# Decayed keys and normalised rows turned on VectorE and by transfers, in place of TensorE

## The reference

```
f = 1 / (1 + exp(-f_logit))
for t in range(S):
    state = f[t, :, None] * state + outer(k[t], v[t])
    y[t] = q[t] @ state
x = y as 3072 rows of 384
xn = x / sqrt(mean(x * x) + 1e-6) * rms_g
x = (silu(xn @ w_gate) * (xn @ w_val)) @ w_out         # hidden width 1536
h = x @ w_in                                           # hidden width 2048
g = h if h >= 1; 0 if h <= -1; else (h + 1)^2 / 4
out = g @ w_out2
```

## Time and profile before

| | |
|---|---|
| median of 3 runs | 984.48 us (984.31 to 984.51) |
| profiled execution | 984.23 us, span 982.5 us |
| busy: TensorE, its weight load, VectorE, ScalarE, GpSimd | 966.8, 943.4, 585.9, 341.8, 22.4 us |
| chain that ended last | TensorE 95%, VectorE 3%, issue 1% |
| slices of the span at a granted clock below 0.9 | none |
| transfers | 42.32 MB in 15774 packets |

### The profile page before, as it was taken

One profiled execution on the slowest core, in us unless ns is written; L12 is line 12 of the kernel. 1 busy time (PEld: TensorE's weight loads), 2 busy tenths in 40 slices (PEclk: granted clock), 3 DMA queues, 4 the chain that ended last, 5 costly groups with the idle time before them and its releaser, 6 DMA issues.

```text
span 982.5 us, 20662 instructions
## 1 busy us (share of the span) xinstructions
PE 966.8 (98%) x8227; PEld 943.4 (96%) x8227; DVE 585.9 (60%) x1196; ACT 341.8 (35%) x624; POOL 22.4 (2%) x58
## 2 busy tenths in 40 slices
PE   6899999999999999999999999999999999999998
PEld 6899999999999999999999999999999999999998
DVE  8778665574674765665565565555545554545454
ACT  2343322322322222223224454344344344434433
POOL 0100000000000000000000000000000000000000
PEclk9999999999999999999999999999999999999999
DMA  5541111011120110111120400000000000000000
GB/s 194 190 149 43 40 42 50 32 48 40 40 71 9 61 52 13 68 40 40 40 87 17 136 27 1 25 0 24 0 24 0 24 0 19 5 5 19 0 25 25
DMA packets 15774, 42.32 MB, mean 43 GB/s; under 512 B 1408, under 2 KB 8064, under 8 KB 15744
## 3 DMA queue, kind: packets, MB, share of 16 engines
q1 hardware_dynamic: 15744, 41.88, 12.5%
HBM read 37.16 MB, written 4.72 MB: 43 GB/s over the span
## 4 chain that ended last, share of the span: by engine, by line
PE 95%; DVE 3%; issue 1%; POOL 0%; ACT 0%; DMA 0%; DVEq 0%; POOLq 0%
PE gate_ps L403 15%; PE val_ps L403 15%; PE acc L479 13%; PE gate_ps L467 10%; PE val_ps L467 10%; PE acc L425 10%; PE acc L483 7%; PE acc L429 5%; PE tb L314 2%; PE y_ps L338 2%; PE y_ps L344 2%; PE tb L324 1%; DVE qd L721 1%; PE ta L300 1%; DVE after L700 1%
## 5 line engine op out<-in xcount | busy, mean ns | idle before, releaser
L837 DVE TENSOR_TENSOR h_lo<-h_buf,h_hi 128x384 fp32r<-128x384 f32 x224 | 123.3, 551 | 13.2 <-ACT h_hi L648 6.2
L641 ACT ACTIVATE act_buf<-act_buf,half_col 128x384 f32<-128x384 f32 x128 | 78.8, 615 | 140.5 <-DVE act_buf L887 140.5
L479 PE MATMUL acc<-h_hi,w_hi 128*128 128x384 f32 x381 | 127.5, 335 | 0.0
L479 PE MATMUL acc<-h_hi,w_lo 128*128 128x384 f32 x381 | 127.4, 334 | 0.0
L584 ACT ACTIVATE act_buf<-gate_ps 128x384 f32<-128x384 f32 x96 | 47.2, 492 | 177.1 <-PE gate_ps L403 177.1
L589 ACT ACTIVATE h_hi<-h_buf 128x384 fp32r<-128x384 f32 x96 | 50.5, 526 | 167.6 <-DVE h_buf L832 167.6
L403 PE MATMUL gate_ps<-x_hi,w_hi 128*128 (+1 forms) x288 | 99.2, 344 | 1.0 <-issue 0.6
L425 PE MATMUL acc<-h_hi,w_hi 128*128 128x384 f32 x288 | 99.1, 344 | 0.0
L403 PE MATMUL val_ps<-x_hi,w_hi 128*128 (+1 forms) x288 | 99.1, 344 | 0.0
L403 PE MATMUL gate_ps<-x_hi,w_lo 128*128 (+1 forms) x288 | 96.5, 335 | 0.0
L403 PE MATMUL val_ps<-x_hi,w_lo 128*128 (+1 forms) x288 | 96.4, 335 | 0.0
(11 more groups left out here) (117 smaller groups left out, 1989.3 us busy)
## 6 DMA issues: line engine op xcount, KB each, us to landing
raw<-qkf_dram SPq DMA_DIRECT2D x21, 768.0 KB, 4.3
x<-wb_dram SPq DMA_DIRECT2D x12, 576.0 KB, 5.2
v_sb<-v_dram SPq DMA_DIRECT2D x24, 192.0 KB, 2.8
out_dram<-x SPq DMA_DIRECT2D x7, 576.0 KB, 2.8
raw<-wc_dram SPq DMA_DIRECT2D x7, 384.0 KB, 3.1
x<-qkf_dram SPq DMA_DIRECT2D x2, 768.0 KB, 6.8
kd<-wc_dram SPq DMA_DIRECT2D x3, 384.0 KB, 3.1
qd<-wc_dram SPq DMA_DIRECT2D x3, 384.0 KB, 3.9
```

What stands on the lines that cost most here:

```text
L479: pe.matmul(acc[:, m, 0:N], wc_part(w, j, 1, m), h_hi[:, j % 2, :], start=(j == 0 and w is w_hi), stop=False)
L641: nc.scalar.activation(act_buf[:, j % 2, :], act_buf[:, j % 2, :], ACT.Square, bias=half_col[:, :], scale=0.5).then_inc(square_ready, 1)
L837: nc.vector.tensor_tensor(h_lo[:, j % 2, :], h_buf[:, j % 2, :], h_hi[:, j % 2, :].bitcast(F32), ALU.subtract).then_inc(done, 1)
```

## The change

In the 21 chunks behind the prologue TensorE no longer turns anything.

- VectorE transposes `kd` (`block_kd`) and `xs` (`block_x`) in blocks of 32 by 32. Each block is turned in place, in its own 32 partitions.
- SP issues 16 transfers for each of the two (`move_kd`, `move_x`), every one carrying four or three blocks from one group of 32 partitions to another. They go from buffers that are free at that time (`after`, `decayed`) to `kdT` and to a part of `scores`.
- The state update takes `kdT` in groups of 32 columns: 16 matmuls instead of 8. ScalarE and VectorE read the turned rows from SBUF, not from PSUM.
- Offsets move: `square_sum` from 11 to 10, `normalise` from 12 to 11 with `block_x` behind it, `decay_state` from 5 to 6, rounding and rest of the rows from 14 to 15. `block_kd` stands ahead of `decay_q` at 3. `turn_kd`, `copy_kdT` and `turn_x` are gone from the slots.
- Buffers that a transfer reads or fills are guarded by new waits: `decay_after` for `kdT_loaded`, `decay_state` for `xT_loaded`, `mask_scores` for `x_lo_ready`.

```diff
+        after = after_words[:, :, 1:C + 1]
+        kd_blocks = after_words[:, 0:NB, 0:C]
-        kdT = sb("kdT", [P, NP, PR])
+        kdT = sb("kdT", [P, NB, NP, BS])
+        xT = scores[:, 0, 0:KM, :].rearrange("f k t -> f (k t)").rearrange("f (a k t) -> f a k t", a=NB, k=KM)
+        x_blocks = decayed[:, :, :].rearrange("p a e -> p (a e)")
...
 
+                def move_kd(n):
+
+                    sp.wait_ge(kd_blocks_ready, n - (CT - 1))
+                    sp.wait_ge(update_made, n)
+                    for a in range(NB):
+                        for b in range(NB):
+                            sp.dma_start(kdT[b * BS:(b + 1) * BS, a, :, :].rearrange("t p d -> t (p d)"),
+                                         kd_blocks[a * BS:(a + 1) * BS, b, :]).then_inc(kdT_loaded, 16)
+
+                def move_x(n):
+
+                    sp.wait_ge(x_blocks_ready, n - (CT - 1))
+                    sp.wait_ge(x_lo_ready, n)
+                    blocks = x_blocks.rearrange("t (b m) -> t b m", b=NB)
+                    for a in range(NB):
+                        for b in range(NB):
+                            sp.dma_start(xT[b * BS:(b + 1) * BS, a, :, :].rearrange("f k t -> f (k t)"),
+                                         blocks[a * BS:(a + 1) * BS, b, :]).then_inc(xT_loaded, 16)
+
                 def load_wb(j):
                     s = CT + j % STAGES
...
                 load_wb(8)
+                move_kd(CT)
                 sp.wait_ge(qd_ready, CT + 1)
                 load_raw(CT + 1)
                 load_wb(9)
                 sp.wait_ge(y_made, 2 * CT + 2)
                 load_v(CT + 1)
                 load_wb(11)
-                with sp.Fori(CT + 2, NCH) as n:
-                    sp.wait_ge(qd_ready, n)
-                    load_raw(n)
-                    sp.wait_ge(y_made, n * 2)
-                    load_v(n)
+                move_x(CT)
+                with sp.Fori(CT + 1, NCH - 1) as n:
+                    move_kd(n)
+                    sp.wait_ge(qd_ready, n + 1)
+                    load_raw(n + 1)
+                    sp.wait_ge(y_made, n * 2 + 2)
+                    load_v(n + 1)
+                    move_x(n)
+                move_kd(NCH - 1)
+                move_x(NCH - 1)
                 stages = len(wc_stages)
                 sp.wait_ge(qd_ready, NCH)
                 for j in range(JC):
                     if j == 2:
                         sp.wait_ge(y_made, 2 * NCH)
+                    if j == stages - 1:
+                        sp.wait_ge(x_lo_ready, NCH)
                     if j >= stages:
...
                     pe.wait_ge(v_loaded, 16 * (n + 1))
-                    pe.wait_ge(kdT_ready, n + 1)
+                    if isinstance(n, int) and n < CT:
+                        pe.wait_ge(kdT_ready, n + 1)
+                    else:
+                        pe.wait_ge(kdT_loaded, (n - (CT - 1)) * MOVED)
                     pe.wait_ge(scores_ready, 2 * n + 1)
                     for p in range(NP):
-                        for r in range(2):
-                            mm = pe.matmul(tb[r * HP:r * HP + D, p * D:(p + 1) * D], kdT[:, p, r * HP:r * HP + D],
-                                           v_sb[:, r, p, :], start=True, stop=True)
+                        for a in range(NB):
+                            m = min(BS, a // 2 * HP + D - a * BS)
+                            mm = pe.matmul(tb[a * BS:a * BS + m, p * D:(p + 1) * D], kdT[:, a, p, 0:m],
+                                           v_sb[:, a // 2, p, :], start=True, stop=True)
                     mm.then_inc(update_made, 1)
 
...
                         o = slot - WINDOW * c
-                        if o == 4:
-                            turn_kd(n, c)
-                        elif o == 6:
+                        if o == 6:
                             score(n, c)
                         elif o == 9:
                             update(n)
                             attend(n, c, 0)
                             attend(n, c, 1)
-                        elif o == 13:
-                            turn_x(n)
 
                 def keep_warm(count):
...
-                def round_x(i, c, bank=tb):
+                def round_x(i, c, bank=None):
                     n = i * CT + c
-                    act.wait_ge(xT_made, n + 1)
-                    if c == 0 and bank is tb:
+                    if bank is None:
+                        act.wait_ge(xT_loaded, (n - (CT - 1)) * MOVED)
+                        rows = xT.rearrange("f a k t -> f k a t")
+                    else:
+                        act.wait_ge(xT_made, n + 1)
+                        rows = bank[:, 0:KM * P].rearrange("p (k t) -> p k t", k=KM)
+                    if c == 0 and bank is None:
                         act.wait_ge(out_made, (i - 1) * JB + 1)
-                    nc.scalar.activation(x_hi[:, i % 2, :, c * C:(c + 1) * C],
-                                         bank[:, 0:KM * P].rearrange("p (k t) -> p k t", k=KM),
-                                         ACT.Copy).then_inc(x_hi_ready, 1)
+                    at = x_hi[:, i % 2, :, c * C:(c + 1) * C]
+                    if bank is None:
+                        at = at.rearrange("f k (a t) -> f k a t", a=NB)
+                    nc.scalar.activation(at, rows, ACT.Copy).then_inc(x_hi_ready, 1)
...
                             sigmoid_f(n)
-                        elif o == 5:
-                            copy_kdT(n)
-                        elif o == 11:
+                        elif o == 10:
                             square_sum(n)
-                        elif o == 14:
+                        elif o == 15:
                             round_x(i, c)
 
...
+                def block_kd(n, c):
+                    dve.wait_ge(kd_ready, n + 1)
+                    dve.wait_ge(whole_made, n + 1)
+                    nc.vector.transpose(kd_blocks.rearrange("d b (p t) -> d p b t", p=NP),
+                                        kd[:, c % 2, :, :].rearrange("d p (b t) -> d p b t", b=NB))\
+                        .then_inc(kd_blocks_ready, 1)
+
+                def block_x(n):
+                    dve.wait_ge(xs_ready, n + 1)
+                    nc.vector.transpose(x_blocks.rearrange("t (b k f) -> t k b f", b=NB, k=KM),
+                                        xs[:, :].rearrange("t (k b f) -> t k b f", k=KM, b=NB))\
+                        .then_inc(x_blocks_ready, 1)
...
                         elif o == 3:
+                            block_kd(n, c)
                             decay_q(n, c)
-                        elif o == 5:
+                        elif o == 6:
                             decay_state(i, c)
                         elif o == 7:
                             mask_scores(n, 0)
                             mask_scores(n, 1)
                         elif o == 9:
                             update_state(n)
-                        elif o == 12:
+                        elif o == 11:
                             normalise(n)
-                        elif o == 14:
+                            block_x(n)
+                        elif o == 15:
                             rest_x(i, c)
 
                 def split_wb(j):
```

More of the change, by code:

```diff
@@ L45 @@
 NW = JB * WB
+BS = 32
+NB = P // BS
+MOVED = 16 * NB * NB
 SLOTS = 3 * JB
@@ L155, in build @@
         x_lo_ready = sem("x_lo_ready")
+        kd_blocks_ready = sem("kd_blocks_ready")
+        kdT_loaded = sem("kdT_loaded")
+        x_blocks_ready = sem("x_blocks_ready")
+        xT_loaded = sem("xT_loaded")
         gate_made = sem("gate_made")
@@ L299, in turn_kd @@
                     for p in range(NP):
-                        mm = pe.transpose(ta[:, p * PR:(p + 1) * PR], kd[0:PR, c % 2, p, :], ident[0:PR, 0:PR])
+                        mm = pe.transpose(ta[:, p * P:(p + 1) * P], kd[:, c % 2, p, :], ident[:, :])
                     mm.then_inc(kdT_made, 1)
@@ L307, in score @@
                         pe.wait_ge(state_ready, n)
-                    if not first:
+                    if not first and isinstance(n, int) and n == CT:
                         pe.wait_ge(x_lo_ready, n)
-                    pe.wait_ge(kdT_ready, n + 1)
+                    if first:
+                        pe.wait_ge(kdT_ready, n + 1)
+                    else:
+                        pe.wait_ge(kd_ready, n + 1)
+                        pe.wait_ge(state_ready, n)
                     for p in range(NP):
@@ L697, in decay_after @@
                         dve.wait_ge(kd_ready, n)
+                    if not isinstance(n, int) or n > CT:
+                        dve.wait_ge(kdT_loaded, (n - CT) * MOVED)
                     for p in range(NP):
@@ L741, in decay_state @@
                         dve.wait_ge(y_made, n * 2)
+                    if not isinstance(n, int) or n > CT:
+                        dve.wait_ge(xT_loaded, (n - CT) * MOVED)
                     if c > 0:
@@ L751, in mask_scores @@
                     dve.wait_ge(scores_made, n + 1)
```

(12 more changed lines are left out.)

17 lines of the change are left out of this document (11 added, 6 removed).

## The result

The changed kernel takes 1186.76 us (median of 4 runs, 1186.29 to 1187.05) against 984.5: ratio 1.205, 95% interval 1.203 to 1.207. The direction was forecast, the size was not: +202 us where +38 was expected, far outside 1001 to 1046.

What follows compares the result with a forecast made beforehand. TensorE was taken as the bound, busy 69.15 of 69.15 us a tile. First tile +13.9, six tiles 24 and prologue 0.2 gave +38 on 984.23: 1022 us, range 1001 to 1046.

Steps and rivals of the forecast that it cites:

- I take 0.40: SP's issues of 32 partitions: 0.40 us each, bounds 0.16 to 0.48, so a move of 16 takes 7.9 us.
- The end-of-tile wait: Next tile's first gate projection waits 2.3 us for the third chunk's moved rows; tile +4.0.
- The keys of the second chunk: Landing at 213.0 behind 32 issues, against an update at 212.52 + 1.3: just covered; 1.6 late at 0.48.
- a sign that it is wrong: Prediction wrong if the tile period is under 69.15, or if the largest wait is on the keys.
- Rounding and rest of the first and second chunk's rows: They delay the next gate products, which still end before TensorE asks: cost nothing.
- Rival 4: TensorE's clock falls to 1.2 GHz in the new waits: 13 to 25 us over eight, 1035 to 1047; chance 0.05.
- Spared on TensorE: Per chunk, rows 0.33, keys 0.40 and update 0.16: 0.89 us, 18.7 in all; 2.67 a tile.
- 0.60 and 0.45 forecast: VectorE's two added transposes, 128x512 and 128x384: 0.60 and 0.45 us, 1.05 per chunk.
- Rival 1: Issues cost 0.16, no end-of-tile wait; VectorE's delays 1.6 a tile and 7.5 in the first: 1001; chance 0.20.
- the order's part of the sum: VectorE's added work ahead of TensorE's products delays attention's end by 1.9, less 0.33: 1.6 us a tile.
- Pass 0: First tile, where SP's queue also carries weights: waits for keys 2.3, gate projection +11.2, +13.9 us in all.
- Rival 3: VectorE's transposes fit its slack, below about 0.2 us together, issues under 0.3: faster, 973; chance 0.05.

Runs made afterwards that it cites:

- Filled waits: The changed kernel with never-read matmuls into a free bank ahead of TensorE's waits for kdT and x_lo: 1164.8 us, 22 less than the change.

## Why the prediction was wrong, point by point

- **The step that failed: "I take 0.40", bounds 0.16 to 0.48, for the issue interval.** Measured 0.63. The earlier trace rows hold only loads from HBM, and I bounded a transfer from SBUF to SBUF by their rows and bytes, which change nothing from 16 to 128 partitions; the route was no term of mine. A move takes 11.3 us, not 7.9.
- The end-of-tile wait: 2.3 forecast, 6.35 measured, 4 more for a move 3.4 longer. The keys of the second chunk, "just covered" behind 32 issues: 4.41, as 32 x 0.23 is 7.4 us later. Those of the first, thought covered, 1.90; those of the third, which my list left out, 2.26. Over the whole execution the keys are the largest wait (54.0 and the 12.1 of pass 0), which the prediction had named as a sign that it is wrong.
- Rounding and rest of the first and second chunk's rows: "nothing" forecast. They hold VectorE, and TensorE waits 2.3 a period more.
- **Rival 4 was not a rival but came on top.** I gave the clock 0.05 as an alternative. It costs 7.0 us a period, behind the second chunk's keys and at the tile's end. Filled waits give back 3.6.
- Spared on TensorE: 2.67 a period forecast, 69.15 - 67.57 = 1.6 measured; keys and update alone 69.15 - 67.75 = 1.4 of 1.68. The update of 32 entries took 0.36 (0.34 forecast).
- VectorE: 0.61 to 0.63 and 0.50 start to start (0.60 and 0.45 forecast). Rival 1, in which only this is left, was 1001 with 1.6 a tile; with a quarter of the transfers it was 1007.5 with 1.9. So the order's part of the sum held for a tile, partly by luck: TensorE was spared 1.1 less than forecast, and the waits for VectorE were 0.8 smaller.
- Pass 0: +13.9 forecast. The first gate projection of the second and of the last tile, in the kernel before and in the changed one:

```profile
105.85 0.33 PE L403 MATMUL gate_ps<-x_hi,w_hi 128*128 128x384 f32 x1
...
520.79 0.33 PE L403 MATMUL gate_ps<-x_hi,w_hi 128*128 x1
```

```profile
146.13 0.66 PE L446 MATMUL gate_ps<-x_hi,w_hi 128*128 128x384 f32 x1 [5.13 <-issue]
...
720.83 0.68 PE L446 MATMUL gate_ps<-x_hi,w_hi 128*128 x1 [6.28 <-DVE x_lo L865]
```

Pass 0 brings +40, the six passes 160 in place of 24, and 2 come behind the last wait.

- Rival 3, faster: its threshold of 0.2 us for VectorE's work was for the places that the change chose. Other places do gain, for the keys alone.

## What to carry to other kernels

Price a transfer by a row of the same route, source and destination both; if the trace has none, the range must be wide, and the count of transfers multiplies it. Where the sum has a wait of two us or more, it needs a second term for the clock behind it, with a range. And before a small gain is judged, look for waits with no releaser at a loop's first instruction: moving code can cost more than the change earns.

## What the runs showed that was not expected

- One issue on SP: 0.63 us SBUF to SBUF, 0.46 between SBUF and HBM either way, 0.70 HBM to HBM, with no effect of 16 to 128 partitions or 64 to 512 bytes in one run each; 0.64 on ScalarE's queue, 0.56 on GpSimd's, side by side with SP's.
- One store of 256 KB to HBM and four gathering loads beat sixteen transfers within SBUF: 1014.8 against 1186.8 us.
- The lower clock (0.50) behind waits of 4.41 and 6.35 us, not behind 1.90 and 2.26 in the same tile; but in other kernels behind 2.45, and not behind 2.54.
- 1.7 to 2.2 us at a jump back of a loop, made and unmade by where it begins.
